# Second layer of a fused attention and feed-forward kernel as seven products of halves instead of eight

## The reference

```python
def _attn_ref(q, k, v, cap):               # q, k, v: (4, 12, 448, 64)
    scores = (1.0 / np.sqrt(64)) * np.matmul(q, k.transpose(0, 1, 3, 2))
    scores = cap * np.tanh(scores / cap)
    attn = np.exp(scores - np.max(scores, axis=-1, keepdims=True))
    attn = attn / (np.sum(attn, axis=-1, keepdims=True) + 1e-09)
    return np.matmul(attn, v)

def _moe_ref(x, w_in, w_out, s, b):        # x: (1792, 768), w_in: (768, 2048), w_out: (2048, 768)
    r = np.maximum(x @ w_in, 0.0)
    g = s * (r * r) + b
    return g @ w_out
```

## Time and profile before

| | us |
|---|---|
| runs of the kernel before | 619.89, 618.86, 758.1 (median 619.89) |
| the profiled execution | 619.69 |
| its span in the trace | 617.9 |
| TensorE busy in the span | 611.7 |
| VectorE, ScalarE, GpSimd busy | 322.0, 290.5, 50.5 |

### The profile page before, as it was taken

One profiled execution on the slowest core, in us unless ns is written; L12 is line 12 of the kernel. 1 busy time (PEld: TensorE's weight loads), 2 busy tenths in 40 slices (PEclk: granted clock), 3 DMA queues, 4 the chain that ended last, 5 costly groups with the idle time before them and its releaser, 6 DMA issues.

```text
span 617.9 us, 8317 instructions
## 1 busy us (share of the span) xinstructions
PE 611.7 (99%) x3218; PEld 483.9 (78%) x3218; DVE 322.0 (52%) x549; ACT 290.5 (47%) x330; POOL 50.5 (8%) x47
## 2 busy tenths in 40 slices
PE   8999999999999999999999999999999999999998
PEld 4335667777787877787779999999888888888998
DVE  4986999975585575585544222223622233221431
ACT  7985776775666676667524222223411232112320
POOL 0114966200000000000000000000000000000000
PEclk9999999999999999999999999999999999999999
DMA  8432445322222222231114221131622233111501
GB/s 298 137 122 59 137 159 174 110 73 92 87 78 88 92 73 92 88 91 43 46 57 147 59 68 52 51 114 41 191 70 68 55 125 112 49 44 36 163 1 65
DMA packets 32103, 57.27 MB, mean 93 GB/s; under 512 B 3584, under 2 KB 18240, under 8 KB 32064
## 3 DMA queue, kind: packets, MB, share of 16 engines
q1 hardware_dynamic: 32064, 56.74, 29.0%
HBM read 40.21 MB, written 16.52 MB: 92 GB/s over the span
## 4 chain that ended last, share of the span: by engine, by line
PE 93%; DVE 2%; ACT 2%; issue 1%; DMA 1%; SPq 0%; ACTq 0%; DVEq 0%
PE banks L527 13%; PE banks L529 13%; PE banks L528 13%; PE banks L539 12%; PE banks L541 12%; PE banks L540 12%; PE banks L472 8%; PE banks L428 5%; PE banks L494 2%; PE banks L452 1%; DMA work<-w_in 1%; PE banks L374 1%; DVE e_sum L800 1%; ACT e L702 1%; ACT e L679 1%
## 5 line engine op out<-in xcount | busy, mean ns | idle before, releaser
L527 PE MATMUL banks<-x_hi,w_hi 128*128 128x448 f32 x384 | 142.6, 371 | 0.0
L529 PE MATMUL banks<-x_hi,w_lo 128*128 128x448 f32 x384 | 140.4, 366 | 0.0
L528 PE MATMUL banks<-x_lo,w_hi 128*128 128x448 f32 x384 | 140.3, 365 | 0.0
L540 PE MATMUL banks<-x_lo,w_hi 128*128 128x512 f32 (+2 forms) x384 | 139.4, 363 | 0.0
L539 PE MATMUL banks<-x_hi,w_hi 128*128 128x512 f32 (+2 forms) x384 | 139.4, 363 | 0.0
L541 PE MATMUL banks<-x_hi,w_lo 128*128 128x512 f32 (+2 forms) x384 | 139.4, 363 | 0.0
L723 ACT ACTIVATE x_hi<-e,beside 128x512 fp32r<-128x512 f32 (+1 forms) x48 | 36.2, 763 | 112.6 <-PE banks L541 112.6
L527 PEld LDWEIGHTS banks<-x_hi,w_hi 128*128 128x128 f32 x384 | 72.1, 188 | 20.3 <-issue 14.0
L904 DVE TENSOR_TENSOR x_lo<-e_sum,x_hi 128x512 fp32r<-128x512 f32 (+1 forms) x48 | 30.0, 626 | 98.8 <-ACT x_hi L723 97.6
L541 PEld LDWEIGHTS banks<-x_hi,w_lo 128*128 128x128 f32 x384 | 72.1, 188 | 9.0
L539 PEld LDWEIGHTS banks<-x_hi,w_hi 128*128 128x128 f32 x384 | 72.1, 188 | 8.9
(11 more groups left out here) (72 smaller groups left out, 595.9 us busy)
## 6 DMA issues: line engine op xcount, KB each, us to landing
hidden_scratch<-hidden_sb SPq DMA_DIRECT2D x48, 224.0 KB, 1.9
beside<-q_k SPq DMA_DIRECT2D x23, 448.0 KB, 3.9
e<-hidden_scratch SPq DMA_DIRECT2D x32, 256.0 KB, 2.7
e<-w_out SPq DMA_DIRECT2D x16, 384.0 KB, 3.1
work<-w_in SPq DMA_DIRECT2D x22, 256.0 KB, 5.5
v_sb<-v SPq DMA_DIRECT2D x24, 192.0 KB, 2.8
y_t<-beside SPq DMA_DIRECT2D x10, 256.0 KB, 2.9
e<-hidden_scratch SPq DMA_DIRECT2D x16, 160.0 KB, 2.2
```

What stands on the lines that cost most here:

```text
L527: nc.tensor.matmul(out, w_hi[:, j, w], x_hi[:, batch % 2, c, :], start=c == 0, stop=False)
L528: nc.tensor.matmul(out, w_hi[:, j, w], x_lo[:, batch % 2, c, :], start=False, stop=False)
L529: last = nc.tensor.matmul(out, w_lo[:, j, w], x_hi[:, batch % 2, c, :], start=False, stop=c == CT - 1)
L540: nc.tensor.matmul(out, w_hi[:, j, w], ring(x_lo, n), start=False, stop=False)
```

## The change

The second layer is computed by a scheme of Strassen's kind (seven products instead of eight). w_out is cut in halves both ways (8 by 3 tiles each), and g in upper and lower halves of its features, and in batches: a pair is batches 0 and 1, or 2 and 3. For each pair seven products of an 8 by 3 tile part with 8 g tiles of 448 tokens are made in place of eight. A step is one product of one pair: 14 steps (`STEPS`) of 8 tiles (`HALF`) and 3 column tiles (`ACCS`) by three matmuls. The steps alternate between the pairs, and each pair has three PSUM banks.

- **Sums of operands.** Products 2 to 5 take sums of w_out's quarters (`s_scratch`); products 3 to 6 sums of g's (`t_scratch`). GpSimd makes them in 24 groups (`COMBINED`): 8 of w_out, 8 for each pair. A group is: SyncE loads two DMAs into `work` (each 128 x 896 or 128 x 768), GpSimd does four dependent tensor_tensor operations of 448 or 384 columns, SyncE stores two DMAs. `work` holds one group: a load waits for the landing of the store before. In slots p = 10 to 23 one group is loaded at the end of each slot and stored behind the next slot's first hidden store; in the last 16 hidden tiles there is one group in four tiles, and in the second layer one in eight.
- **Sums of products.** ScalarE copies products 0 and 2 out (`copy_out`, 12 copies); VectorE adds the others (`add_up`): 3 operations in a step of products 1 and 6, 6 in a step of 3, 4 and 5, each of 448 columns.
- **g.** Hidden tiles of batch 3 go through DRAM too. 14 x 8 = 112 tiles are split, not 64. For the first 64 (`BIASED`) VectorE has two operations, for the others one, since s(r1 - r2) has no b. RING is 6, in places of 448.
- **w_out.** 28 loads and splits of 2 x 384 columns (7 products by 4), in four buffers.
- **Order.** The first layer's last 16 tiles are no longer mixed with second-layer products; these follow.

```diff
+HALF = JT // 2
+HALF_DM = DM // 2
+ACCS = HALF_DM // P
+PRODUCTS = 7
+HALVES = B // 2
+STEPS = PRODUCTS * HALVES
+LAST = STEPS * HALF
+BIASED = 4 * HALVES * HALF
+RING = CT
...
+W_TILES = 2
+W_STEPS = HALF // W_TILES
+W_BUFFERS = JT // (HALF // 2)
+COMBINED = ([(-1, k) for k in range(6)] + [(0, k) for k in range(HALF)] + [(-1, k) for k in range(6, HALF)]
+            + [(1, k) for k in range(HALF)])
+COMBINE = PAIRS + 4
...
+            def combine_load(m):
...
+                    sp.wait_ge(w_in_lo, PIECES)
+                else:
+                    sp.wait_ge(combine_out, 32 * m)
...
+                for half in range(2):
+                    j = half * HALF + k
+                    if pair < 0:
+                        sp.dma_start(work_flat[:, half * DM:(half + 1) * DM], w_out[j * P:(j + 1) * P, :]
+                                     ).then_inc(combine_in, 16)
+                    else:
+                        sp.dma_start(work_flat[:, half * 2 * S:(half + 1) * 2 * S],
+                                     hidden[j, :, pair * 2 * S:(pair + 1) * 2 * S]).then_inc(combine_in, 16)
+            def combine_store(m):
+                pair, k = COMBINED[m]
+                sp.wait_ge(combine_done, m + 1)
+                for half in range(2):
+                    if pair < 0:
+                        sp.dma_start(s_sums[half, k], work_flat[:, half * DM:(half + 1) * DM]).then_inc(combine_out, 16)
+                    else:
+                        sp.dma_start(t_sums[half, k, :, pair * 2 * S:(pair + 1) * 2 * S],
+                                     work_flat[:, half * 2 * S:(half + 1) * 2 * S]).then_inc(combine_out, 16)
...
+                reach(sp, w_out_hi, m - W_RAW + 1)
+                reach(sp, w_out_lo, m - W_RAW + 1)
...
+                    for of in range(t * W_TILES, (t + 1) * W_TILES):
+                        sp.wait_ge(combine_out, 32 * (COMBINED.index((-1, of)) + 1))
...
+                    source = s_sums[half, tiles, :, column:column + HALF_DM].rearrange("k p n -> p k n")
+                sp.dma_start(w_out_raw[:, m % W_RAW], source).then_inc(w_out_in[m % W_RAW], 16)
...
+                reach(sp, g_hi_done, n - RAW + 1)
+                reach(sp, g_lo_done, n - RAW + 1)
...
+                else:
+                    sp.wait_ge(combine_out, 32 * (COMBINED.index((pair, k)) + 1))
+                    source = t_sums[1 if i in (3, 6) else 0, k, :, first:first + S]
+                sp.dma_start(raw(n), source).then_inc(hidden_in[n % RAW], 16)
...
+                    if p > COMBINE and j == tiles_beside(batch - 1, c).start:
+                        combine_store(p - COMBINE - 1)
+                if p >= COMBINE:
+                    combine_load(p - COMBINE)
...
+            sp.wait_ge(pv_done, products(ALL - 1))
...
+            for m in range(W_RAW):
+                load_w_out(m)
+            for n in range(RAW):
+                load_g(n)
+            combined = ALL - COMBINE - 1
             for j in range(JT):
...
-                    sp.wait_ge(pv_done, products(ALL - 1))
-                    sp.wait_ge(e_sum_done, 3 * ALL)
-                reach(sp, w_out_hi, j - W_RAW + 1)
-                reach(sp, w_out_lo, j - W_RAW + 1)
-                sp.dma_start(w_out_raw[:, j % W_RAW, :], w_out[j * P:(j + 1) * P, :]).then_inc(w_out_in[j % W_RAW], 16)
...
-            for i in range(3):
-                sp.wait_ge(hidden_out[i], 16 * ((B - 1) * JT // 3))
-            for n in range((B - 1) * JT):
...
-                reach(sp, g_hi_done, JT + n - RAW + 1)
-                reach(sp, g_lo_done, JT + n - RAW + 1)
-                first, width = TOKENS[n // JT + 1]
-                sp.dma_start(raw(n), hidden[n % JT, :, first:first + width]).then_inc(hidden_in[n % RAW], 16)
-                if n % JT == RAW + 1:
...
+                store_hidden((B - 1) * JT + j)
+                if W_STEPS < j <= 2 * W_STEPS:
+                    load_w_out(W_RAW + j - W_STEPS - 1)
+                if j % 4 == 1:
+                    combine_store(combined + j // 4)
+                if j % 4 == 2:
+                    combine_load(combined + j // 4 + 1)
+            combined += JT // 4
+            for n in range(RAW, LAST):
+                load_g(n)
+                m, off = divmod(n - RAW - RING - 1, W_STEPS)
+                m += W_RAW + W_STEPS
+                if off == 0 and m < W_STEPS * PRODUCTS:
+                    load_w_out(m)
+                if n % HALF == 6 and combined < len(COMBINED):
+                    combine_store(combined)
+                    combined += 1
+                if n % HALF == 0 and n > HALF and combined < len(COMBINED):
+                    combine_load(combined)
+                step = step_at(n - RAW - 1)
+                if step is not None and step // HALVES in (1, 4, 5):
+                    store_y(step)
+            for step in (STEPS - 2, STEPS - 1):
+                store_y(step)
...
-            def out_product(order, j, c):
...
-                nc.tensor.matmul(out, w_hi[:, j, w], ring(x_hi, n), start=j == 0, stop=False)
-                nc.tensor.matmul(out, w_hi[:, j, w], ring(x_lo, n), start=False, stop=False)
-                last = nc.tensor.matmul(out, w_lo[:, j, w], ring(x_hi, n), start=False, stop=j == JT - 1)
...
+            def out_product(step, k, d):
+                i, pair = divmod(step, HALVES)
+                n = step * HALF + k
+                out = acc(pair, d)
+                if k == 0:
...
+                    if i == 1:
+                        pe.wait_ge(p_copied, pair * ACCS + d + 1)
+                    elif i == 2:
+                        pe.wait_ge(c11_done, pair * ACCS + d + 1)
...
+                    elif i == 4:
+                        pe.wait_ge(u2_done, pair * ACCS + d + 1)
...
+                nc.tensor.matmul(out, w_tile(w_hi_flat, i, k, d), ring(x_hi, n), start=k == 0, stop=False)
+                nc.tensor.matmul(out, w_tile(w_hi_flat, i, k, d), ring(x_lo, n), start=False, stop=False)
+                last = nc.tensor.matmul(out, w_tile(w_lo_flat, i, k, d), ring(x_hi, n), start=False, stop=k == HALF - 1)
...
+            for chunk in range(CT * JT):
+                hidden_chunk(B - 1, chunk)
+            for step in range(STEPS):
+                for k in range(HALF if step < STEPS - 1 else HALF - 2):
+                    out_ready(step, k)
+                    for d in range(ACCS):
+                        out_product(step, k, d)
...
+            def w_out_high(m):
+                act.wait_ge(w_out_in[m % W_RAW], 16 * (m // W_RAW + 1))
+                free_w_place(act, m)
+                nc.scalar.copy(w_place(w_hi_flat, m), w_out_raw[:, m % W_RAW]).then_inc(w_out_hi, 1)
+            def g_high(n):
...
+                if n < RING:
...
+                    act.wait_ge(hid_done, (B - 1) * JT)
...
+                    act.wait_ge(out_used, n - RING + 1)
+                if n < BIASED:
+                    nc.scalar.activation(ring(x_hi, n), raw(n), ACT.Identity, scale=s_c, bias=b_c).then_inc(g_hi_done, 1)
...
+                    nc.scalar.activation(ring(x_hi, n), raw(n), ACT.Copy, scale=s_c).then_inc(g_hi_done, 1)
...
+            def copy_out(step):
+                i, pair = divmod(step, HALVES)
+                for d in range(ACCS):
+                    acc_complete(act, step, d)
+                    place = second_sum(pair, d) if i else first_sum(pair, d)
+                    nc.scalar.copy(place, acc(pair, d)).then_inc(p_copied, 1)
...
-            def square(n):
...
-                nc.vector.scalar_tensor_tensor(r, r, s_c, r, ALU.mult, ALU.mult).then_inc(sq_done, 1)
-            def low_of(source, n):
...
+            def w_out_low(m):
+                dve.wait_ge(w_out_hi, m + 1)
+                nc.vector.tensor_tensor(w_place(w_lo_flat, m), w_out_raw[:, m % W_RAW], w_place(w_hi_flat, m).bitcast(F32),
+                                        ALU.subtract).then_inc(w_out_lo, 1)
+            def g_low(n):
+                if n < BIASED:
...
-                    dve.wait_ge(hidden_in[(n - JT) % RAW], 16 * ((n - JT) // RAW + 1))
-                    nc.vector.tensor_scalar(g_tile(n), source, s_c, b_c, ALU.mult, ALU.add).then_inc(g_done, 1)
+                    dve.wait_ge(hidden_in[n % RAW], 16 * (n // RAW + 1))
+                    nc.vector.tensor_scalar(g_tile(n), raw(n), s_c, b_c, ALU.mult, ALU.add).then_inc(g_done, 1)
                 dve.wait_ge(g_hi_done, n + 1)
...
+                if n < BIASED:
+                    dve.wait_ge(g_done, n + 1)
                     nc.vector.tensor_tensor(ring(x_lo, n), g_tile(n), ring(x_hi, n).bitcast(F32), ALU.subtract
                                             ).then_inc(g_lo_done, 1)
...
                 else:
...
+                    nc.vector.scalar_tensor_tensor(ring(x_lo, n), raw(n), s_c, ring(x_hi, n).bitcast(F32),
+                                                   ALU.mult, ALU.subtract).then_inc(g_lo_done, 1)
+            def add_up(step):
```

(53 more changed lines are left out.)

285 lines of the change are left out of this document (168 added, 117 removed).

## The result

The changed kernel takes 598.62 us (median of 4 runs, 597.92 to 600.41) against 619.89 us for the kernel before in the same sitting: a ratio of 0.9666, 95% interval 0.9644 to 0.9688. One of the four runs of the kernel before took 758.1 us, a slow one, and is left out of its median and of the ratio. The forecast was 593.3 us. So the sign is right, the time lies in the forecast's range (591.5 to 604), and 5.3 us are missing: of the 26.6 us predicted, 21.3 arrived. The profiled execution took 600.41 us (span 598.6).

A forecast was written before the change was run, and what follows sets the result against it. TensorE's matmuls were taken to bound the kernel: 619.69 us for the profiled execution, -26.9 for matmuls, +0.3 for the tail, other costs 0, gives 593.1; the median run stands 0.2 above, so 593.3 us, range 591.5 to 604.

The forecast's parts named there:

- The matmul term: Second layer on TensorE: 1008 matmuls of 448 columns, 204.3 us, replace 231.2 us of matmuls: -26.9 us.
- One eighth less: Plain estimate for the second layer's matmuls, 28.9 us saved; the prediction rejected it as too much, by 2 us.
- Tail: End of the kernel: last VectorE operation +0.14 us for 448 columns, last store +0.17 us for 64 KB more: +0.3 us.
- Slots: First layer, slots 10 to 23: SyncE stands 3 us each time, within 11 us of slack; cost taken as 0.
- DMA rate: Second-layer step with a group: 4.5 MB in 14.6 us, 305 GB/s, under 377; cost taken as 0.
- GpSimd beside VectorE: Second layer: a group holds VectorE at most 4.4 us, in seven of 14 steps; cost taken as 0.
- rival 2: Second layer: VectorE, held by GpSimd, loses its lead; 7 us lost, 600 us; chance 0.18 together with rival 1.
- The loop through DRAM: Group loads, four GpSimd operations, stores through `work`: 14.9 us, 14.5 in the mean, against rounds of 15.2, later 14.6; cost 0.
- rival 1: SyncE falls behind in the DRAM loop each time; 11 us lost at a 16.2 us loop, 604 us; chance 0.18 with rival 2.
- The slack: Raw-tile loads in the second layer: issued 12.8 us ahead, landing in 2.7 us, so some 9 us for SyncE's delays.
- lead of 7.7 us for VectorE: Second layer: the ring of six gives five tiles, 9.1 us, less 1.4 us latency of VectorE and ScalarE; cost taken as 0.
- The case given 0.70: The forecast itself, 593.3 us for the whole kernel, with no loss above 2 or 3 us; chance 0.70.

The follow-up runs named there:

- two_places: The changed kernel with a second buffer from group 14 on, each group loaded before the one ahead is stored: 593.5 us, ratio 0.9579; again 593.19 us, 0.9575.
- dma_only: The changed kernel with the groups' loads and stores kept and GpSimd's sums left out: 593.18 us, ratio 0.9571 to the kernel before.
- gpsimd_only: The changed kernel with GpSimd's operations kept and the groups' loads and stores left out: 593.72 us, ratio 0.9584 to the kernel before.
- one_split: The changed kernel with scale and bias put on hidden tiles by a third ScalarE operation, leaving VectorE one subtraction a tile: 599.28 us, ratio 0.9671.
- second run: The changed kernel, unchanged, measured again in the sitting of the experiments: 599.59 us, ratio 0.9674 to the kernel before.

## Why the prediction was right, and where it wasn't

- **The matmul term** (-26.9 us): right to the fourth digit. Without groups, and in two_places, 1007 distances have a mean of 0.2027 us. That 0.2027 was read from the kernel before at 448 columns, and not scaled from 512, is what made it exact. "One eighth less" would have been 2 us off.
- **Tail** (+0.3): measured +0.36 (3.46 us behind the last matmul's start against 3.10).
- **Slots** (0): right, with SyncE's waits of 2.8 us for a forecast of 3.
- **DMA rate** (305 GB/s): measured 302, and harmless: dma_only.
- **GpSimd beside VectorE.** The forecast counted 4.4 us of holding a step and "0.8 us of lead lost in a step, with 7.7 to lose". The Trainium skill, page "SBUF — State Buffer", section "Who interferes with whom", which the forecast cites for two-input operations, also names tensor_scalar among those that can take the ports shared with GpSimd. The forecast passed over this: its argument against rival 2 counts one-input operations as free of the effect. The trace agrees with the page: the one-input operation goes from 0.51 to 1.35 us. In the mean a biased tile takes VectorE 0.76 + 0.69 us for 0.63 + 0.51, 0.31 us more or 2.5 us a step of eight, inside the 4.4 us. By itself it costs nothing: gpsimd_only.
- **The step that failed: "The loop through DRAM ... I take 0".** The loop turned out at 15.5 us (group loads at 372.40 and 481.15, seven loops apart) for a forecast of 14.5 to 14.9, against a round of 14.6. Its parts can be read in the timelines of SyncE and GpSimd, as means of the seven loops: from the load's issue to GpSimd's start 5.1 us (forecast 5.1), the four operations 5.5 (forecast 6.1), 0.02 to the store's issue, and from there to the next load 4.9 (forecast 3.7). The term that was mis-sized is that of the two stores: ahead of each of the seven next loads SyncE waits for their landing, the later of which took 3.5 to 6.1 us. This is rival 1's mechanism. But by rival 1's own formula, 11 (15.5 - 14.6) - 9, such a loop costs 1 us at most, since it leaves 9 us of slack to be used up first.
- **The slack was the other half.** "12.8 - 2.7 = some 9 us" (the subtraction gives 10.1) used a landing measured with the DMA engines 27% busy. At 88% it is 4.8 us, and the slack 8.0. And at the start there is none: tile 7 is issued 5.8 us before TensorE wants it, behind the group's load, which the forecast's order of the tiles passed over. The forecast's lead of 7.7 us for VectorE goes there, in one wait of 8.0 us, and VectorE, busy 94 of 103 us, can't win it back; with spare time it can, as one_split shows. So rival 2's mechanism, a VectorE without a lead, is what turned a loop late by 1 us a round into 5 us.
- **The chances.** The case given 0.70, no loss above 2 or 3 us, did not come: 5.3 us were lost. What came is rivals 1 and 2 together, which had 0.18, and their range, up to 604, held the time. The total is near because the loss is small beside the matmul term, not because the loop was rightly priced.
- **What no step had:** a stop can cost more than its own length. About 2 of the 8 us in the profiled execution are matmuls 0.2067 us apart behind a stop.

## What to carry to other kernels

A queue that issues in order must not wait for another engine's product between the loads that feed the bottleneck: load one group ahead into a second buffer, and the same work costs nothing (here a ratio to the kernel before of 0.9579 and 0.9575, against 0.9666 and 0.9674). Count the slack of a prefetch with the landing time under the load that the change brings, and count from where the load really stands in the order, at the first tile as well as in the steady state. Two resources that are each 90% full may each be harmless, as two runs show here, and still leave no room to make up for a third thing that comes late.

## What the hardware showed that was not expected

- After a stop of TensorE, its matmuls of 448 columns may run 0.2067 us apart and not 0.2027 at the same granted clock of 1.00, to the end of the layer, 180 us on. In the changed kernel the wider distance ended at tile 40, behind a further stop. The length of a stop doesn't decide: behind the 2.1 us at tile 7 the changed kernel went on at 0.2027, behind the 0.5 us at the same tile its second run went on at 0.2067. What sets it stays open: which stops switch it on, and why. The two runs with a stop put in show only that a stop can do it.
- VectorE's tensor_scalar with one SBUF input, 448 columns of fp32, takes 0.51 us alone and up to 1.35 beside a GpSimd operation with two inputs. The forecast had counted it as free of that.
- Full DMA engines double the landing of a 224 KB load without costing TensorE anything, as long as loads are issued in time: between 397 and 500 us a raw tile landed in 6.1 us in dma_only (0.88 of the 16 engines busy, 309 GB/s) and in 3.1 in gpsimd_only (0.63, 197 GB/s), and TensorE was busy throughout in both.
